# Two banks for the value sums, and q and k turned and hashed through one bank in halves

## What is computed

```python
q_bits = (np.einsum('bhsd,dk->bhsk', q, proj) > 0)      # 6 bits; k_bits likewise
mask = q_bucket[:, :, :, None] == k_bucket[:, :, None, :]
scores = np.where(mask, scale * np.matmul(q, k.transpose(0, 1, 3, 2)), -1000000000.0)
attn = np.exp(scores - np.max(scores, axis=-1, keepdims=True))
attn = attn / (np.sum(attn, axis=-1, keepdims=True) + 1e-09)
x = np.matmul(attn, v)                                   # B, H, S, D = 2, 8, 768, 64
h = np.maximum(np.maximum(x @ w1, x @ w2), x @ w3)       # 1536 x 512 by 512 x 768
x = h @ w_out
h = x @ w_in                                             # 512 x 2048
return np.where(h > 0, h, np.exp(np.minimum(h, 0)) - 1) @ w_out2
```

## Time and profile before

| | |
|---|---|
| median of three runs | 746.4 us |
| the profiled execution | 744.61 us, span of its records 742.8 us |
| TensorE busy | 720.6 us (97%) |
| its granted clock, mean | 0.989 |
| VectorE, ScalarE, GpSimd busy | 380.8, 424.5, 367.8 us |
| attention | from 0 to about 280 us of the span |

### The profile page before, as it was taken

The page is one execution under the profiler, slowest core; times in us unless marked ns, Lnnn a source line. Parts: engine busy times, 40 slices in busy tenths (PEclk is TensorE's granted clock), DMA queues, the critical chain, the costliest instruction groups (busy, mean ns, idle before and its releaser), DMA issues.

```text
span 742.8 us, 10492 instructions
## 1 busy us (share of the span) xinstructions
PE 720.6 (97%) x3469; PEld 618.8 (83%) x3469; DVE 380.8 (51%) x615; ACT 424.5 (57%) x821; POOL 367.8 (50%) x333
## 2 busy tenths in 40 slices
PE   6899999999999979999999999999999999999998
PEld 5699999999998868888888888788888888888886
DVE  6768888988888844322222221243344433444333
ACT  4488989989898982221222121355555555555553
POOL 5377888888888871021110010254545444454442
PEclk8799999999999999999999999999999999999999
DMA  7656456464545000211000010133334333343331
GB/s 150 156 112 137 97 129 146 92 135 97 123 107 136 0 1 21 65 43 44 21 22 1 21 34 31 54 104 98 89 111 143 102 97 94 105 142 108 92 100 56
DMA packets 79317, 63.44 MB, mean 85 GB/s; under 512 B 29080, under 2 KB 68712, under 8 KB 79272
## 3 DMA queue, kind: packets, MB, share of 16 engines
q1 hardware_dynamic: 77416, 62.47, 33.0%
q10 hardware_dynamic: 1856, 0.40, 0.3%
HBM read 40.91 MB, written 3.15 MB: 59 GB/s over the span
## 4 chain that ended last, share of the span: by engine, by line
PE 60%; DVE 0%; ACT 0%; issue 0%
PE banks L781 14%; PE banks L783 14%; PE banks L782 14%; PE banks L1128 6%; PE banks L1124 6%; PE banks L1125 6%; DVE g_sb L1067 0%; DVE g_sb L1063 0%; DVE out_sb L1037 0%; ACT gh L1022 0%; ACT neg L1017 0%
## 5 line engine op out<-in xcount | busy, mean ns | idle before, releaser
L934 POOL TENSOR_TENSOR wl<-raw,wh 128x512 fp32r<-128x512 f32 (+2 forms) x104 | 143.5, 1398 | 301.7 <-ACT wh L950 301.7
L351 POOL TENSOR_TENSOR p_lo<-probs,p_hi 128x384 fp32r<-128x384 f32 x192 | 197.0, 1043 | 53.9 <-ACT p_hi L419 53.0
L781 PE MATMUL banks<-xh,wh 128*128 128x512 f32 x408 | 158.9, 389 | 0.5 <-PEq L126 0.5
L782 PE MATMUL banks<-xl,wh 128*128 128x512 f32 x408 | 158.8, 389 | 0.0
L783 PE MATMUL banks<-xh,wl 128*128 128x512 f32 x408 | 158.7, 389 | 0.0
L556 DVE TENSOR_REDUCE half_max<-banks 128x1 f32<-128x384 f32 x192 | 99.5, 547 | 27.7 <-PE banks L677 26.8
L418 ACT ACTIVATE probs<-banks 128x384 f32<-128x384 f32 x192 | 95.1, 495 | 26.2 <-PE banks L692 22.5
L419 ACT ACTIVATE p_hi<-banks 128x384 fp32r<-128x384 f32 x192 | 95.1, 496 | 0.0
L1063 DVE TENSOR_SCALAR g_sb<-banks 128x512 f32<-128x512 f32 x48 | 33.2, 692 | 120.1 <-ACT neg L1017 120.1
L781 PEld LDWEIGHTS banks<-xh,wh 128*128 128x128 f32 x408 | 76.6, 188 | 17.0 <-issue 0.9
L783 PEld LDWEIGHTS banks<-xh,wl 128*128 128x128 f32 x408 | 76.5, 188 | 16.0
(11 more groups left out here) (119 smaller groups left out, 1189.4 us busy)
## 6 DMA issues: line engine op xcount, KB each, us to landing
operands<-wh SPq DMA_DIRECT2D x36, 384.0 KB, 7.0
raw<-in_moe_w_in SPq DMA_DIRECT2D x48, 256.0 KB, 2.7
raw<-in_moe_w_out SPq DMA_DIRECT2D x48, 256.0 KB, 2.8
raw<-in_moe_w SPq DMA_DIRECT2D x18, 256.0 KB, 3.9
wl<-wh SPq DMA_DIRECT2D x9, 384.0 KB, 6.7
v_raw<-in_v SPq DMA_DIRECT2D x16, 192.0 KB, 2.5
out_dram<-out_sb SPq DMA_DIRECT2D x12, 256.0 KB, 2.1
q_raw<-in_q SPq DMA_DIRECT2D x15, 192.0 KB, 3.4
```

Source lines behind the costliest of these rows:

```text
L351: pool.tensor_tensor(p_lo[:, at, :], probs[:, step % RING, :], p_hi[:, at, :].bitcast(FP32), ALU.subtract).then_inc(pl_done, 1)
L781: pe.matmul(out, sh, mh, start=first, stop=False)
L782: pe.matmul(out, sh, ml, start=False, stop=False)
L934: pool.tensor_tensor(wl[:, j, at:at + cols], raw[:, j, at:at + cols], wh[:, j, at:at + cols].bitcast(FP32), ALU.subtract).then_inc(w_ready, 1)
```

## The change

The value sums get two banks, one per half of the queries. The second comes from `misc`, which shrinks to one bank (`single`) after the first slots. So q and k are turned three tiles (half) at a time: after the three transposes of one half, ScalarE copies its high part (`high_half`, 384 columns) and VectorE subtracts to get its low part (`low_half`, 384 columns), and only then may the next three transposes overwrite the bank. There are now four such groups in an odd slot, in steps 0, 3, 5 and 8 (`TP_AT`), where there were two, of six transposes, in steps 0 and 6. The hash of k goes through the same bank as that of q and waits for q's bits. The hardware loop is gone: its slots are written out. Slots -3 to 0 turn and hash as before.

```diff
-TP_AT, HASH_AT = (0, 6), (3, 6)
+TP_AT, HASH_AT = ((0, 3), (5, 8)), (3, 6)
+LOW_AT = ((4, 7), (11, None))
...
-        pv_ps = banks[:, RING + 2, :]
+        pv_ps = [banks[:, RING + 2 + i, :] for i in range(2)]
         misc = banks[:, RING + 3:, :]
+        single = banks[:, RING + 4, :]
...
+            def high_half(s, x, n, half):
+                if half == 0:
+                    act.wait_ge(t_half, s.count(1, n - 1))
+                else:
+                    act.wait_ge(t_ready, s.count(1, 3 + n))
...
+                act.activation(hi[x][:, half, :], single[:, 0:HALF], ACT.Copy
+                               ).then_inc(hi_done if half else hi_half, 1)
...
-                    if s.has_tp and step == TP_AT[0] + 1:
+                    if s.has_tp and s.off <= FIRST_SLOT + 2 and step == 1:
                         high(s, "q", 1)
+                    for i, name in enumerate("qk"):
+                        if s.has_tp and s.off > FIRST_SLOT + 2 and step - 1 in TP_AT[i]:
+                            high_half(s, name, i + 1, TP_AT[i].index(step - 1))
...
+            def low_half(s, x, n, half):
+                if half == 0:
+                    dve.wait_ge(hi_half, s.count(1, n - 1))
+                else:
+                    dve.wait_ge(hi_done, s.count(1, 3 + n))
+                dve.tensor_tensor(lo[x][:, half, :], single[:, 0:HALF], hi[x][:, half, :].bitcast(FP32), ALU.subtract
+                                  ).then_inc(lo_done if half else lo_half, 1)
...
+                    for i, name in enumerate("qk"):
+                        if s.has_tp and s.off > FIRST_SLOT + 2 and n in LOW_AT[i]:
+                            low_half(s, name, i + 1, LOW_AT[i].index(n))
...
+            def transposes_half(s, x, n, half):
+                src = q_raw if x == "q" else k_raw
+                par = (s.off + 3) // 2 % 2
+                if half == 1:
+                    pe.wait_ge(lo_half, s.count(1, n - 1))
+                elif n == 1:
+                    pe.wait_ge(q_in[par], s.count(8, 56 - 16 * par))
+                    pe.wait_ge(bits_done, s.count(1, 3))
+                else:
+                    pe.wait_ge(k_in[par], s.count(8, 56 - 16 * par))
+                    pe.wait_ge(lo_done, s.count(1, 4))
+                for t in range(TH):
+                    last = pe.transpose(single[:, t * P:(t + 1) * P],
+                                        src[:, par, half * TH + t, :, :].rearrange("p a d -> p (a d)"), ident[:])
+                last.then_inc(t_ready if half else t_half, 1)
...
+                if s.off > FIRST_SLOT + 3 and n == 2:
+                    pe.wait_ge(bits_done, s.count(1, 3))
...
-                    wait(pe, o_read, s.count(4, -2 if step < LAG else 0))
+                    wait(pe, o_read, s.count(4, -4 if step < LAG else -2))
...
-                out, kept = pv_ps[:, 0:HALF], (STEPS * s.off + step - LAG) % KEPT
+                half = at // T
+                out, kept = pv_ps[half][:, 0:HALF], (STEPS * s.off + step - LAG) % KEPT
```

More of the change, by code:

```diff
@@ L99, with all_slots @@
     has_hash = property(lambda s: not s.odd and -2 <= s.off <= HEADS - 4)
-def all_slots(eng, emit):
-    for s in range(FIRST_SLOT, LOOP_FROM):
+def all_slots(emit):
+    for s in range(FIRST_SLOT, LAST_SLOT + 1):
         emit(Slot(s))
[L106 to L115, removed]
 def wait(eng, sem, count):
-    if not isinstance(count, int) or count > 0:
+    if count > 0:
         eng.wait_ge(sem, count)
@@ L266, in emit @@
                 if s.has_max:
-                    head = held(sp, s.count(1, 1))
+                    head = s.count(1, 1)
                     wait(sp, vl_done, s.count(1))
@@ L371, in outcome @@
                 act.wait_ge(pv_ready, s.count(2, half - 1))
-                act.activation(x[rows, unit, :], pv_ps[0:D, 0:HALF], ACT.Copy).then_inc(o_read, 1)
-                act.activation(inv[rows, unit, :], pv_ps[D:P, 0:HALF], ACT.Copy).then_inc(o_read, 1)
+                act.activation(x[rows, unit, :], pv_ps[half][0:D, 0:HALF], ACT.Copy).then_inc(o_read, 1)
+                act.activation(inv[rows, unit, :], pv_ps[half][D:P, 0:HALF], ACT.Copy).then_inc(o_read, 1)
+            def high_half(s, x, n, half):
[3 more added lines that the diff above has]
+                    act.wait_ge(t_ready, s.count(1, 3 + n))
+                for a in range(2):
+                    act.wait_ge(spread1[a], s.count(SPREAD1 / 2, 1.5 * SPREAD1))
+                    act.wait_ge(spread2[a], s.count(SPREAD2 / 2, 1.5 * SPREAD2))
+                act.activation(hi[x][:, half, :], single[:, 0:HALF], ACT.Copy
+                               ).then_inc(hi_done if half else hi_half, 1)
             def high(s, x, n):
@@ L503, in take_bits @@
                 elif x == "q":
-                    last = dve.tensor_scalar(bits[:, 0, :], misc[:, 0, 0:HALF], 0.0, half_bits[:], ALU.is_gt,
+                    bank = misc[:, 0, :] if s.off == FIRST_SLOT + 3 else single
+                    last = dve.tensor_scalar(bits[:, 0, :], bank[:, 0:HALF], 0.0, half_bits[:], ALU.is_gt,
                                              ALU.subtract)
                 else:
-                    last = dve.tensor_scalar(bits[:, 1, :], misc[:, 1, 0:HALF], k_above[:], k_times[:], ALU.is_gt,
+                    last = dve.tensor_scalar(bits[:, 1, :], single[:, 0:HALF], k_above[:], k_times[:], ALU.is_gt,
                                              ALU.mult)
@@ L578, in emit @@
                     low(s, "q", 1)
+                elif s.off == FIRST_SLOT:
+                    low(s, "k", 2)
                 elif s.has_tp:
-                    low(s, "k", 2)
+                    low_half(s, "k", 2, 1)
                 if s.has_max:
@@ L713, in weigh @@
                         pe.wait_ge(empty_done, s.count(1, 1))
-                    half = at // T * HALF
-                    pe.matmul(out, total[:, h % 2, :], empty[:, h % 2, half:half + HALF], start=False, stop=True
+                    pe.matmul(out, total[:, h % 2, :], empty[:, h % 2, half * HALF:(half + 1) * HALF], start=False, stop=True
                               ).then_inc(pv_ready, 1)
@@ L727, in emit @@
                     for i, x in enumerate("qk"):
-                        if s.has_tp and step == TP_AT[i] and s.off != FIRST_SLOT + 2:
+                        if s.off == FIRST_SLOT and step == 6 * i:
                             transposes(s, x, i + 1)
+                        if s.has_tp and s.off > FIRST_SLOT + 2 and step in TP_AT[i]:
+                            transposes_half(s, x, i + 1, TP_AT[i].index(step))
                         if s.off == FIRST_SLOT + 2 and x == "q" and step == 3:
```

38 lines of the change are left out of this document (19 added, 19 removed).

## The result

The changed kernel takes 752.47 us (median of four runs, 751.87 to 753.28) where the kernel before took 746.1 us in the same session; the ratio is 1.0076 (95% interval 1.0056 to 1.0095). Forecast were 749.5 us, a range of 744.0 to 753.5, and slower as the likeliest sign.

What follows compares the result with a forecast made beforehand. TensorE was taken to set the pace up to about 255 us, ScalarE close behind. Odd slots' 11.7 us of waits, less 1.8, 1.2 (even slots) and 5.6 (tail), gave +3.1 on 746.4: 749.5 us, range 744.0 to 753.5.

Steps and rivals of the forecast that it cites:

- The sign and the odd slots: Slower, at 0.58; halves' waits add 1.95 us per odd slot, 11.7 for six, less 1.8 for freed value-bank waits.
- steps 5, 8 and 3: Odd slots: k's first half, k's second and q's second wait 0.82, 0.60 and 0.2 us for round trips over ScalarE and VectorE.
- 0.18 for two more groups of transposes: Odd slots: the first matmul pair behind each group of transposes is 0.09 us slower; two more groups make 0.18.
- The even slots: Freed bank waits mostly stay, as step 3's maxima wait for VectorE; gain 0.2 us each, 1.2 for six (bounds 0, 3.3).
- at nothing: Attention's hardware loop written out: no time gained or lost; extra code is fetched ahead (up to 1 us lost if not).
- The tail: Slots 13 to 16: freed bank waits gain 1.8 us in 13 and 14, 3.8 behind, 5.6 in all (bounds 3.8, 9).
- the forecast's upper bound: Tail: 9 us gained if all waits go at full price and a stretch of half clock goes as well.
- ScalarE pays twice: Odd slots: two copies of 0.81 us become four of 0.53, 0.5 us more, hidden by TensorE's new waits.
- The sum: Whole kernel: 11.7 - 1.8 - 1.2 - 5.6 = +3.1 us, from 746.4 to 749.5 us.
- rival 4: Odd slots: ScalarE's double payment shows, 0.5 us each since it is full there; 752.5 us, chance 0.10.
- Rival 5: Written-out loop: its code is fetched late; 751 us, chance 0.02.

Runs made afterwards that it cites:

- copies first: Changed kernel with all four of ScalarE's copies of a half put ahead of the exponentials of their step: 745.18 us, 0.9989 of before.
- the wide schedule: Kernel with copies first, its four transpose groups in steps 0, 4, 7, 10 instead of 0, 3, 5, 8, low parts moved too: 750.29 us, 1.0052.
- the later reciprocal: Kernel with copies first and split early, VectorE's first reciprocal put one place later, behind maxima 9: 748.18 us, 1.0024 of before.
- one value bank: Changed kernel with both halves of the value sums in one bank again and the old wait for it: 756.32 us, 1.0127 of before.
- split early: Changed kernel with VectorE's 1536-column subtraction (low part of first expert weights, slot 15) put ahead of the value totals: 751.87 us, 1.0081 of before.

## Why the prediction was right, and where not

**The sign and the odd slots: right, and shown.** Forecast were waits of 0.82, 0.60 and 0.2 us in steps 5, 8 and 3 of odd slots, and slots of 16.5 (its sum, 14.99 + 1.95 - 0.3, makes 16.6). In slot 9 of the changed kernel:

```profile
178.54 0.55 PE L686 MATMUL banks<-ident,q_raw 128*128 128x128 f32 x3
...
182.08 0.52 PE L686 MATMUL banks<-ident,k_raw 128*128 128x128 f32 x3 [0.70 <-DVE wh L502]
...
186.26 0.33 PE L686 MATMUL banks<-ident,k_raw 128*128 128x128 f32 x1 [0.33 <-DVE wh L502]
```

By starts the three cost 0.29, 0.86 and 0.50 us over the pace, and the slot lasts 16.47. Those of steps 5 and 8 are what the forecast said: a chain of scores, exponentials, copy and subtraction against a fixed number of matmuls, in which the subtraction starts 0.03 us behind its copy. Moving q's copy took 0.72 of step 5's 0.86 and left step 8's, and moving all took step 8's whole.

Step 3's was near its forecast by luck. The forecast made it a chain through ScalarE's copy, with 0.04 us from the copy to the subtraction. But the subtraction starts 0.21 behind the copy, held by a reduction in VectorE's queue, and with the copy 0.76 us earlier against it (0.97) the transposes are exactly as late. VectorE's order is the limit there, which the forecast had not looked at. The forecast's 0.18 for two more groups of transposes is not there either: from the first transposes of q to the second matmul behind them it is 0.83 us for six and 0.50 for three (174.52 to 175.02 in the changed kernel), and two such threes, less the one matmul's distance of 0.17 that is then counted twice, make 0.83 again.

**The even slots: wrong, in sign.** The step of the forecast that failed was "I take 0.2 us for each of six even slots, 1.2 us (bounds 0 and 3.3)". They lost 0.21 us each instead (16.00 to 16.21), 1.3 in all. That the maxima of step 3 would take the place of the freed wait was right: with the halves' copies moved, even slots with two banks (16.05) equal those with one bank and no halves, written out (16.06), so the second bank gives 0.0, the lower bound. What I had left out is the copy of k's second half in step 9. ScalarE waits for TensorE just ahead of it, then has copy and exponentials to do together, and comes to the next slot 0.16 us late; v's copy, v's low part and the maxima follow (ScalarE, VectorE, TensorE in the changed kernel, slots 9 and 10; the last matmul shown is the one of maxima 5, in step 3, 0.46 us behind the one ahead of it):

```profile
188.13 0.49 ACT L420 ACTIVATE probs<-banks 128x384 f32<-128x384 f32 x1 [0.99 <-PE banks L731]
188.89 0.50 ACT L374 ACTIVATE wh<-banks 128x384 fp32r<-128x384 f32 x1
...
192.87 0.53 ACT L429 ACTIVATE v_hi<-v_raw 128x384 fp32r<-128x384 f32 x1
...
193.42 0.93 DVE L557 TENSOR_TENSOR v_lo<-v_raw,v_hi 128x384 fp32r<-128x384 f32 x1 [0.20 <-ACT v_hi L429]
...
194.28 1.01 DVE L574 TENSOR_REDUCE half_max<-banks 128x1 f32<-128x384 f32 x2
...
194.88 0.44 PE L716 MATMUL banks<-operands 96*128 96x384 f32 x1
```

Moving that copy alone gave back 0.16 of the 0.21: v's copy, v's low part and that matmul come 0.15 to 0.17 us earlier. The rest is what the slots lost when they were taken out of the loop (16.00 to 16.06), which I had put at nothing.

**The tail: right mechanism, half the size.** Forecast 5.6 us: 1.8 in slots 13 and 14 and 3.8 behind. From before to the changed kernel the two slots gave 0.85 and the tail 1.84, 2.7 in all. For the slots the forecast had looked at the room of ScalarE and GpSimd only (1.2 and 1.6 us). The freed time of step 6 runs into the maxima of step 7, which wait for VectorE:

```profile
248.15 0.34 PE L748 MATMUL banks<-p_hi,v_lo 128*64 128x384 f32 x1
248.83 0.44 PE L716 MATMUL banks<-operands 96*128 96x384 f32 x1 [0.34 <-DVE half_max L574]
```

Behind them I had priced GpSimd's tiles at 1.0 us each without looking at what VectorE does beside them, although has three of them in 3.96 us. Moving the subtraction gave 1.5 us, which leaves the tail 0.5 short of the 3.8; what that is was not told apart, but GpSimd still loses 1.2 us to the moved subtraction. The stretch of half clock in the tail of before (0.95 mean from 265 to 270 us, 0.71 from 270 to 275) is gone, as the forecast's upper bound had it; the changed kernel has 1.00 from 265 us to the end of the attention.

**ScalarE pays twice: right.** It is busy 15.09 us of the odd slot of 16.42, 0.3 more than before (0.5 forecast) and hidden. With the copies first the odd slot is 15.32, 0.26 over the version with the loop written out and no halves. That it is not ScalarE which holds it there is read from the trace alone: the transposes of steps 3 and 5 start 0.29 and 0.14 us late, behind subtractions that start 0.97 and 0.60 us after ScalarE's copy was done; against that stands the value bank's wait in step 6, 0.3 to 0.4 us in the written-out version, which is gone. No run moved VectorE's subtractions ahead to show it.

**The sum.** With measured terms: odd slots 6 x 1.49 = +8.9, even slots +1.3, slots 13 and 14 -0.85, tail -1.84: +7.5 us. The two profiled executions differ by 7.9, the medians by 6.4: the profiled one of before, at 744.61, was 1.5 us faster than its median. The microsecond between 7.5 and 6.4 is less than what the start varies by: the profile of the changed kernel reached slot 1 2.8 us earlier than the profile of before, and has in that slot a wait of 1.96 us for the hash bits' transfer, and half clock for a stretch behind it (0.89 mean).

```profile
42.21 0.62 PE L716 MATMUL banks<-operands 96*128 96x384 f32 x2 [1.96 <-DMA operands<-bits]
...
41.00:57.00 16.00, 13.73 (x73) 12.57 (x74) 8.74 (x18) 11.29 (x26) 8.81 (x10) 0.89 0.33 77
```

The forecast of +3.1 was thus short by 3.3 in the medians, and by 4.4 in these terms: the even slots account for 2.5 and the tail for 2.9, while the odd ones came out below it (8.9 against 11.7 - 1.8 = 9.9). Two of the three terms that were to pay for the halves failed, one in sign and one by half, and the time stayed inside the range because that reached up to 753.5.

The measured 752.47 is also what rival 4 had (752.5), but not by its mechanism: it wanted 0.5 us more in each odd slot, from a full ScalarE, and the odd slots last 16.48, as forecast. What took the time past the forecast is the even slots and the tail. Rival 5, late code, has nothing for it: written out, the kernel before takes 1.0004 of its time.

## What to carry to other kernels

A buffer split to free another turns one long operation into a chain of round trips; price each as the length of the chain from the last thing that every link waits for, against the work of the waiting engine in between, and look at what stands ahead of each link in its own engine's queue. Putting the link ahead of work that is waiting anyway can be worth more than the buffer: four copies moved by one place were worth 7 us, the second bank 3 to 5. Before counting a wait as gained, ask what the same engine would have waited for next: in the even slots it was a reduction on VectorE that came no earlier, and in step 3 of the odd ones an earlier copy gained nothing, because the subtraction behind it stood behind a reduction. And read such a chain past its own place: the wide schedule lost most in the even slot behind the one that it was made for, and the later reciprocal did nothing for slots 13 and 14 and cost the odd ones 0.85 us, because where it had stood it filled a wait of its engine.

## What was not expected of the hardware

- Slots written out ran up to 0.1 us slower than the same slots in a hardware loop (slot 8: 16.07 against 15.97; slot 9: 15.03 against 14.97), though the program's order is the same. Slot 12 of before lasts 15.97 too, although most of it stands behind the loop. The cause is open.
- A GpSimd subtraction of 384 columns took 2.18 us beside a VectorE subtraction of 1536 columns (1.69 us), and 1.0 us without it.
- The start of the program, up to the turn of slot 0, took 36.62, 41.29 and 41.62 us in the profiles of three kernels with the same work up to there (changed, one value bank, split early). TensorE's clock stood at the lower of its two levels (half) in different stretches of it: for 6.8 us in all in the first, 6.8 in the second and 20.5 in the third, so the clock alone does not make the difference.
